# A fused attention and MLP kernel on one core: pair 0's first contraction a step later, tails transposed by quarters, x1's second piece in the other bank, V's second-group products a step on

## What is computed

```python
def phi(x):
    proj = np.einsum('bhsd,df->bhsf', x, w_phi)
    proj = proj - np.max(np.abs(proj), axis=-1, keepdims=True)
    return np.concatenate([np.exp(proj), np.exp(-proj)], axis=-1)
q_p, k_p = (phi(q), phi(k))                       # q, k, v: (4, 8, 576, 64)
kv = np.einsum('bhsf,bhsd->bhfd', k_p, v)
z = np.sum(k_p, axis=2)
attn = einsum(q_p, kv) / (einsum(q_p, z) + 1e-06)

x = attn as (4, 576, 512)
h = np.maximum(x @ w_in, 0.0)                     # d_ff = 1024
gate = sigmoid(conv of width 3 over the sequence, per channel, of h)
x1 = h * gate @ w_out

u = x1 + (x1.transpose(0, 2, 1) @ U @ V).transpose(0, 2, 1)   # rank 32
out = u + np.maximum(u @ w_ch1, 0.0) @ w_ch2      # 512 -> 2048 -> 512
```

## Time and profile before

| | |
|---|---|
| median of 3 runs | 838.63 us (838.49, 838.63, 840.66) |
| profiled execution | 840.61 us, of which the span is 838.8 us |
| PE busy | 824.2 us, 98% |
| DVE, ACT, POOL busy | 375.5, 295.4, 104.9 us |
| PE's granted clock, mean of the span | 0.996 |

### The profile page before, as it was taken

The page is one execution under the profiler, slowest core; times in us unless marked ns, Lnnn a source line. Parts: engine busy times, 40 slices in busy tenths (PEclk is TensorE's granted clock), DMA queues, the critical chain, the costliest instruction groups (busy, mean ns, idle before and its releaser), DMA issues.

```text
span 838.8 us, 17762 instructions
## 1 busy us (share of the span) xinstructions
PE 824.2 (98%) x7619; PEld 803.3 (96%) x7619; DVE 375.5 (45%) x641; ACT 295.4 (35%) x598; POOL 104.9 (13%) x74
## 2 busy tenths in 40 slices
PE   7999999999999999999999999999999999999997
PEld 5779999999999999999999999999999999999997
DVE  5667883578736786359654421221212212212111
ACT  3675753467434665345333212111112111111111
POOL 1511641003200032004200010100100100000000
PEclk9999999999999999999999999999999999999999
DMA  6756525185232821437535112012001101201101
GB/s 119 179 136 222 179 68 168 35 287 139 82 91 57 289 88 52 177 103 263 194 131 164 51 38 76 1 30 85 1 1 63 51 1 51 63 1 38 38 0 38
DMA packets 99197, 80.75 MB, mean 96 GB/s; under 512 B 63409, under 2 KB 86833, under 8 KB 97073
## 3 DMA queue, kind: packets, MB, share of 16 engines
q1 hardware_dynamic: 98368, 79.44, 31.0%
q10 hardware_dynamic: 752, 0.20, 0.1%
HBM read 61.79 MB, written 17.83 MB: 95 GB/s over the span
## 4 chain that ended last, share of the span: by engine, by line
PE 97%; DVE 1%; ACT 1%; issue 1%; ACTq 0%; DVEq 0%
PE qnb L1119 8%; PE qnb L1117 8%; PE qnb L1118 8%; PE mb L1117 7%; PE mb L1118 7%; PE mb L1119 7%; PE pjb L1119 6%; PE pjb L1117 6%; PE pjb L1118 6%; PE kvb L1124 5%; PE qnb L1124 4%; PE tpb L1117 2%; PE kvb L1119 2%; PE kvb L1117 2%; PE tpb L1119 2%; PE tpb L1118 2%
## 5 line engine op out<-in xcount | busy, mean ns | idle before, releaser
L1038 DVE SCALAR_TENSOR_TENSOR c_lo<-qnb,c_hi 128x384 fp32r<-128x384 f32 x94 | 52.4, 558 | 282.8 <-ACT c_hi L810 282.8
L810 ACT ACTIVATE c_hi<-qnb 128x384 fp32r<-128x384 f32 x94 | 46.3, 492 | 294.3 <-PE qnb L1119 290.4
L1117 PE MATMUL qnb<-u_hi,w_b 128*128 128x384 f32 x384 | 129.7, 338 | 0.0
L1119 PE MATMUL qnb<-u_hi,w_b 128*128 128x384 f32 x384 | 128.4, 334 | 0.0
L1118 PE MATMUL qnb<-u_lo,w_b 128*128 128x384 f32 x384 | 128.4, 334 | 0.0
L548 POOL TENSOR_TENSOR g_lo<-cv,g_hi 128x576 fp32r<-128x576 f32 x31 | 54.0, 1741 | 245.9 <-DVE g_hi L852 238.3
L1118 PEld LDWEIGHTS qnb<-u_lo,w_b 128*128 128x128 f32 x384 | 72.1, 188 | 0.0
L1117 PEld LDWEIGHTS qnb<-u_hi,w_b 128*128 128x128 f32 x384 | 72.1, 188 | 0.0
L1119 PEld LDWEIGHTS qnb<-u_hi,w_b 128*128 128x128 f32 x384 | 72.1, 188 | 0.0
L1117 PE MATMUL mb<-x_hi,winr 128*128 128x288 f32 x224 | 68.4, 306 | 0.1
L1118 PE MATMUL mb<-x_lo,winr 128*128 128x288 f32 x224 | 66.0, 295 | 0.0
(11 more groups left out here) (278 smaller groups left out, 1838.3 us busy)
## 6 DMA issues: line engine op xcount, KB each, us to landing
winr<-wi_dram SPq DMA_DIRECT2D x24, 512.0 KB, 4.9
woutr<-wo_dram SPq DMA_DIRECT2D x11, 1024.0 KB, 5.6
stage<-in_moe_w_ch_dram SPq DMA_DIRECT2D x32, 256.0 KB, 4.1
us<-u_dram SPq DMA_DIRECT2D x6, 768.0 KB, 4.8
ua<-u_dram SPq DMA_DIRECT2D x6, 768.0 KB, 4.7
qr<-in_q_dram SPq DMA_DIRECT2D x32, 128.0 KB, 3.0
vt<-in_v_dram SPq DMA_DIRECT2D x32, 128.0 KB, 3.2
wi_dram<-winr SPq DMA_DIRECT2D x8, 512.0 KB, 3.9
```

The costliest lines, as they stand in the source:

```text
L810: nc.scalar.activation(c_hi[:, j % CR, :], CH[j % 2][:, 0:TW], ACT.Relu).then_inc(s_chh, 1)
L1038: nc.vector.scalar_tensor_tensor(out=c_lo[:, j % CR, :], in0=CH[j % 2][:, 0:TW], scalar=0.0, in1=c_hi[:, j % CR, :].bitcast(F32), op0=ALU. ...
L1117: mm(o, a_hi, b_hi, start=start, stop=False)
L1119: return mm(o, a_lo, b_hi, start=False, stop=stop)
```

## The change

Four edits, all in the order of the work or in the banks that it uses.

1. Pair 0's `K0` contraction moves on PE from tick 2 to tick 3, and ACT computes the exponentials of pair 0's `K0` and `K1` one tick later, behind that tick's copy of transposed data. Other pairs stay.
2. For pairs 0 to 2 (`quartered`) the tail of `at` is transposed by two products of its 64x64 quarters with the identity, which put both heads beside each other in 64 columns; ACT and DVE then take it with one instruction each instead of two. The quarters come before the four full tiles.
3. For batches 0 and 1 the second piece of x1's transposition uses the other bank (`x1_bank`). Group 0's second piece moves from (12, 2) to (12, 1). The waits change with it: the third piece waits for the first, output 4 waits also for the second piece's low part, and group 1's second piece waits for group 0's last addition.
4. V's products of the second group: the first moves from (18, 2) to (19, 0), the second from (19, 0) to (19, 1).

```diff
+    def quartered(g):
+        return PERIOD * g + T_OUT < MLP0 - 1
...
-    X1_AT = {(12, 0): (0, 0), (12, 2): (0, 1), (13, 0): (0, 2),
+    X1_AT = {(12, 0): (0, 0), (12, 1): (0, 1), (13, 0): (0, 2),
              (16, 2): (1, 0), (17, 0): (1, 1), (17, 2): (1, 2)}
...
-             (18, 2): (1, (0,)), (19, 0): (1, (1,)), (19, 2): (1, (2, 3))}
+             (19, 0): (1, (0,)), (19, 1): (1, (1,)), (19, 2): (1, (2, 3))}
...
+    def x1_bank(b, g, i):
+        return 1 - mix_bank(g) if b < B - 2 and i == 1 else mix_bank(g)
...
+        def otail(g):
+            if quartered(g):
+                return [(slice(0, P), OTAIL[:, 0:TAIL])]
+            return [(rows, OTAIL[rows, rows]) for rows in HROWS]
...
-                    for rows in HROWS:
-                        last = copy(x0_hi[rows, g % XS, MAIN:S], OTAIL[rows, rows])
+                    for rows, o in otail(g):
+                        last = copy(x0_hi[rows, g % XS, MAIN:S], o)
...
                 if use is not None:
                     transposed_high(*use)
+                if tick in (K0 + 2, K1 + 2):
+                    key_features(0, tick - 2)
                 g, u = unit_at(tick - 1)
-                if b is None and g is not None and u == K0:
+                if b is None and g and u == K0:
                     key_features(g, u)
...
-                if (b is not None or u != K0) and g is not None and u <= TL:
+                if (b is not None or u != K0) and g is not None and u <= TL and (g or u == TL):
                     key_features(g, u)
...
+                    if quartered(g):
+                        for rows in HROWS:
+                            mm(OTAIL[rows, 0:TAIL], at[rows, g % 2, token_slot(TM), rows], ident[rows, rows], start=True, stop=True)
                     for t in range(TM):
                         last = nc.tensor.transpose(TP[:, t * P:(t + 1) * P], at[:, g % 2, token_slot(t), :], ident[:, :])
-                    last = nc.tensor.transpose(OTAIL, at[:, g % 2, token_slot(TM), :], ident[:, :])
+                    if not quartered(g):
+                        last = nc.tensor.transpose(OTAIL, at[:, g % 2, token_slot(TM), :], ident[:, :])
...
-                    if i and beside(b, g):
+                    if b == B - 2 and i and beside(b, g):
                         pe.wait_ge(s_xml, XP * (2 * b + g) + i)
+                    elif b < B - 2 and i == 1 and g == 1:
+                        pe.wait_ge(s_u, 2 * CC * b + CC)
+                    elif b < B - 2 and i == 2:
+                        pe.wait_ge(s_xml, XP * (2 * b + g) + 1)
...
                         pe.wait_ge(s_ox, 2 * CC * b + (e - 1 if e < 5 else e))
+                        if e == 4 and b < B - 2:
+                            pe.wait_ge(s_xml, XP * 2 * b + 2)
...
-                if b is None and new is not None:
+                if b is None and new:
                     contract_k(new, K0)
...
-                if g is not None and mlp_at(tick - 1)[0] is not None:
+                if g is not None and (g == 0 or mlp_at(tick - 1)[0] is not None):
                     contract_k(g, K0)
```

More of the change, by code:

```diff
@@ L720, in mlp @@
                     if beside(b, g):
-                        x1_high(b, g, i, M[:, mix_bank(g), :])
+                        x1_high(b, g, i, M[:, x1_bank(b, g, i), :])
                 for e, _, last in out_parts(b, m, piece):
@@ L896, in transposed_low @@
                     sub(x0_lo[:, g % XS, 0:MAIN], TP[:, :], x0_hi[:, g % XS, 0:MAIN].bitcast(F32))
-                    for rows in HROWS:
-                        last = sub(x0_lo[rows, g % XS, MAIN:S], OTAIL[rows, rows],
+                    for rows, o in otail(g):
+                        last = sub(x0_lo[rows, g % XS, MAIN:S], o,
                                    x0_hi[rows, g % XS, MAIN:S].bitcast(F32))
@@ L963, in mixing @@
                     if beside(b, g):
-                        x1_low(b, g, i, M[:, mix_bank(g), :])
+                        x1_low(b, g, i, M[:, x1_bank(b, g, i), :])
                 if (m, piece) in TU_AT:
@@ L1331, in mlp @@
                     g, i = X1_AT[m, piece]
-                    if i and beside(b, g):
+                    if b == B - 2 and i and beside(b, g):
                         pe.wait_ge(s_xml, XP * (2 * b + g) + i)
+                    elif b < B - 2 and i == 1 and g == 1:
+                        pe.wait_ge(s_u, 2 * CC * b + CC)
+                    elif b < B - 2 and i == 2:
+                        pe.wait_ge(s_xml, XP * (2 * b + g) + 1)
                     if beside(b, g):
-                        x1_by_token(b, g, i, M[:, mix_bank(g), :])
+                        x1_by_token(b, g, i, M[:, x1_bank(b, g, i), :])
                 for e, first, last in out_parts(b, m, piece):
```

## The result

| | before | changed |
|---|---|---|
| median, runs of the first measurement | 838.56 us (4 runs, 838.20 to 840.66) | 833.53 us (4 runs, 833.19 to 834.13) |
| profiled execution | 840.61 us, span 838.8 | 833.51 us, span 831.7 |
| PE busy | 824.2 us, 98% | 821.2 us, 99% |
| PE's granted clock, mean | 0.996 | 0.998 |

The ratio is 0.9921, 95% interval 0.99 to 0.9941: faster by more than the noise. On the 838.6 us of before that is 832.0 us (830.2 to 833.7), where I had forecast 834.2, with 832.3 to 836.2. So the sign was right and the gain was larger than I said: 5.0 us between the medians and 7.1 between the two profiled executions, against 4.4 and 5.8.

The account below looks back on a forecast made before the run. TensorE, busy 824.2 of 838.8 us, was taken as the bound, so only its waits could be won. Gains of 1.8 + 0.6 + 2.0 = 4.4 us from 838.6 gave 834.2 us, range 832.3 to 836.2.

Parts of the forecast that it names:

- Part 1: Pair 0's start: K0's contraction one step later fills PE's idle gap; 1.8 us on the median, 3.2 against the profiled run.
- The basis: Kernel before: clock fall near 10 us in some runs only; forecast taken from its 838.6 us median, gain 4.4, not 5.8.
- Rival 1: Start: the clock fall was in the median run and goes, the 2.0 offset being the profiler's; gain 5.8, 832.8 us; chance 0.22.
- parts 3 and 4: Mixing, batches 0 and 1: x1's second piece in the other bank, V's second-group products later; 2.0 us together, ends 0 and 2.0.
- Part 2: Quartered tails, pairs 0 to 2: shorter path to PE's tail tile, 3 x 0.21 = 0.6 us; ends 0 and 2.1.
- the ACT row's 0.21: Tails of pairs 0 to 2: one ACT copy instead of two shortens ACT's chain before the query contraction by 0.21 us each.
- x1's 1.1: x1's transpositions, batches 0 and 1: four PE waits for DVE's xt_lo, 1.1 us in all, would go.
- my 0.4 for the later products: V's second group, batches 0 and 1: the last product gets its addition in time, 2 x 0.2 = 0.4 us.
- Rival 2: Start: clock falls in the changed kernel, not in the median before; start gains only 0.3 us, 835.7 us; chance 0.13.
- Rival 3: Mixing: waits only move on to output 4 or hidden's first step; parts 3 and 4 give nothing, 836.2 us; chance 0.12.
- Rival 4: Start: the second pair's data come after 11.7 us and hold PE about 1.4 us; 835.6 us; chance 0.05.
- Rival 5: Reordered start: too little PE activity keeps the clock at 1.2 GHz far beyond 13.3 us; slower, 841.2 us or more; chance 0.03.

## Why the prediction was right and wrong

The forecast missed by 2.2 us, 834.2 against 832.0. About 0.7 of that is the changed kernel itself, 833.5 against 834.2; the other 1.5 or so is the kernel before, which the ratio puts at 840.2 and I had put at 838.6. Two steps of the prediction failed, one mainly behind each.

**Part 1, against the profiled run: right.** The contraction of K0 came at 10.00 (forecast 10.06) without idle time before it, K1's at 12.26 (12.3), the clock stayed at 1.00 at the start, and the gain was 3.29 (3.2). Against a run whose clock did not fall there the timeline has 1.81 (1.8). The medians show 1.0 to 1.3 of it; where the rest of the 1.8 goes is open.

**The basis: the first step that failed.** "So I make the sum for both", and then the sum for the median, 4.4, became the whole forecast. The observation under it was right: the fall of the clock is in some runs and not in others. What I put at nothing is what those runs weigh. The upper level as a whole is 42 of 93, at least 27 of them with the fall, and none of the 10 runs of the changed kernel is there. The mean of before is 840.0, 1.3 above its lower level, that of the changed kernel 833.75: 6.3 us. That the median of my few runs lay at the lower level was partly luck, since in one set of 35 it did not. Rival 1 (832.8 us) had the wrong mechanism, an offset of the profiler's, and the right consequence, that the fall counts. The ratio gives 832.0, beyond rival 1 as well, since parts 3 and 4 were also too small; and the low end of my range, 832.3, left only 0.5 below that rival. How much of the upper level goes by part 1 and how much is the second cause's is not shown.

**Part 2: right.** 0.6 forecast, 0.50 in the timeline, 0.5 in the medians. The waits for x_lo went from 0.69 to 0.29, more than the ACT row's 0.21, but the contraction of queries then began late by ACT's chain, as said.

**Parts 3 and 4: the second step that failed.** "Parts 3 and 4: 1.1 + 0.5 + 0.4 = 2.0. Ends: 0 ... and 2.0, all that stands there": the mechanism was right, the size and above all the upper end were not. The waits went and did not come back; the runs gave 3.10 in the timeline (x1 0.50, 0.45, 0.49 and 0.48; V 0.59 twice), and about 2.8 to 3.1 in the medians. A wait of 0.27 in a matmul's row costs 0.48 to 0.51, as putting the waits back showed (2.0 for four), so the mis-sized term is x1's 1.1, which is 2.0. For V the weight loads' rows had 0.9 where I took 0.5; with my 0.4 for the later products that is 1.3, against 1.18 read. That this is V's cause was not tried apart. The sum with these rows would have been 1.8 + 0.6 + 2.0 + 1.3 = 5.7 us, 832.9 on 838.6, with 833.5 measured.

**The rivals.** Rival 2 (clock falls in the changed kernel only): none of 34 runs with part 1 has a clock under 0.998, and none of the five profiles shows the fall at the start. Rival 3 (waits move on): no such wait in the mixing. Rival 4 (data late): not in the changed kernel's two profiles, once in the kernel with the waits put back. Rival 5: in none of the five profiles.

## What to carry to other kernels

An idle time that a busy engine's matmul rows show in front of a wait is a lower bound: read the weight loads' row too, and the distance from an instruction before to one behind the wait, with the wait and without; its price is the difference, here 0.49 for a shown 0.27, and the weight loads' row had 0.5. Before a gain is forecast from a median, look whether the runs lie at two levels, and ask of the change whether it removes the upper one, since that counts in every mean. Read the clock by stretches: a run's mean of 0.998 stood both for a fall that cost time and for one behind the last matmul. Here a gap of 2.0 us at the start was worth filling with work that was only waiting behind it in the engine's own order.

## What was not expected of the hardware

- An idle gap of 2.0 us on TensorE brings the fall from 2.4 to 1.2 GHz in some executions of one and the same kernel and not in others: at least 27 of 93, whose mean clock is 0.994 to 0.997, and three of the six profiles with the gap. With the gap cut to about 0.85 us, or filled with 1.68 us of products or 1.36 us of transpositions, none of 58 runs has such a mean, and none of seven profiles has the fall at the start.
- A stall named "issue" comes irregularly at 37 to 40 us, in or before a group of small products: 0.30, 0.57, 1.12 and 1.26 us in four of the eight profiles of kernels without part 1 and in none of the five with it. The one shown as 0.30 cost 0.72: in the same group PE takes 1.32 us instead of 0.60. What makes it, and whether part 1 has anything to do with it, stays open.
- A wait that is not yet satisfied costs TensorE more than the idle time at its matmul: at four 128x128 transpositions 0.49 us for an idle 0.27. The overlap of one group's end with the next one's start, 0.16 us, is lost as well, and the group itself takes 0.06 longer.
